# Layer 2's first products by Strassen's scheme: two token tiles and two weight blocks together

## The reference, cut to what matters

```python
h = x @ w_in
g = np.where(h >= 1, h, np.where(h <= -1, 0.0, (h + 1) ** 2 / 4))   # layer 1
x = g @ w_out
h = x @ w_in2                                                       # layer 2
r = np.maximum(h, 0.0)
y = (r * r) @ w_out2
```

## Time and profile before

| what | us |
|---|---|
| median of 3 runs (977.24 to 977.39) | 977.29 |
| span of the profiled execution, first to last instruction | 975.8 |
| what lies around the span, by the median | 1.5 |
| PE busy | 962.4 (99% of the span) |
| DVE busy | 601.0 (62%) |
| ACT busy | 430.9 (44%) |
| POOL busy | 42.0 (4%) |

### The profile page before, as it was taken

One profiled execution on the slowest core, in us unless ns is written; L12 is line 12 of the kernel. 1 busy time (PEld: TensorE's weight loads), 2 busy tenths in 40 slices (PEclk: granted clock), 3 DMA queues, 4 the chain that ended last, 5 costly groups with the idle time before them and its releaser, 6 DMA issues.

```text
span 975.8 us, 22918 instructions
## 1 busy us (share of the span) xinstructions
PE 962.4 (99%) x9520; PEld 781.8 (80%) x9520; DVE 601.0 (62%) x1480; ACT 430.9 (44%) x735; POOL 42.0 (4%) x59
## 2 busy tenths in 40 slices
PE   8899999999999999999999999999999999999998
PEld 7688788777877877787778888888888888888887
DVE  7789888787978787889647763434334334333332
ACT  6667543453455435544545553333333333333333
POOL 5810000000000000000000000000000000000000
PEclk9999999999999999999999999999999999999999
DMA  8252131113012201110004411010010010000000
GB/s 261 81 174 67 59 119 48 27 38 91 35 34 73 71 21 33 49 55 2 2 20 155 162 33 65 1 65 1 1 65 1 0 65 1 33 1 1 33 1 32
DMA packets 28838, 50.65 MB, mean 52 GB/s; under 512 B 2368, under 2 KB 17728, under 8 KB 28736
## 3 DMA queue, kind: packets, MB, share of 16 engines
q1 hardware_dynamic: 28736, 49.19, 15.4%
HBM read 39.75 MB, written 9.44 MB: 50 GB/s over the span
## 4 chain that ended last, share of the span: by engine, by line
PE 87%; DVE 5%; ACT 5%; DMA 2%; issue 1%; SPq 1%; DVEq 0%; ACTq 0%
PE psum L1354 37%; PE psum L1330 37%; PE psum L1077 2%; PE psum L1163 2%; PE psum L1102 1%; PE psum L1214 1%; DVE act_g L1659 1%; ACT kn_sb L804 1%; PE psum L1221 1%; DMA ring<-in_v_s 1%; PE psum L1028 1%; PE psum L1246 1%; ACT act_g L890 1%; DVE diag L1476 1%; ACT u_sb L814 1%
## 5 line engine op out<-in xcount | busy, mean ns | idle before, releaser
L1330 PE MATMUL psum<-x_hi,w 128*128 128x512 f32 x1152 | 390.1, 394 | 0.0
L1354 PE MATMUL psum<-g_hi,w 128*128 128x512 f32 x1152 | 389.7, 393 | 0.0
L1330 PEld LDWEIGHTS psum<-x_hi,w 128*128 128x128 f32 x1152 | 216.1, 188 | 48.9
L1354 PEld LDWEIGHTS psum<-g_hi,w 128*128 128x128 f32 x1152 | 216.1, 188 | 48.4 <-issue 1.8
L1665 DVE TENSOR_TENSOR g_lo<-act_g,g_hi 128x512 fp32r<-128x512 f32 x192 | 132.3, 689 | 159.7 <-ACT g_hi L903 158.6
L1354 PE MATMUL psum<-g_lo,w 128*128 128x512 f32 x576 | 224.3, 389 | 0.0
L903 ACT ACTIVATE g_hi<-act_g 128x512 fp32r<-128x512 f32 x192 | 121.3, 632 | 232.8 <-PE psum L1354 170.6
L1330 PE MATMUL psum<-x_lo,w 128*128 128x512 f32 x576 | 224.0, 389 | 0.0
L1659 DVE TENSOR_TENSOR act_g<-act_g 128x512 f32<-128x512 f32 x96 | 66.4, 691 | 112.1 <-ACT act_g L896 112.1
L1354 PEld LDWEIGHTS psum<-g_lo,w 128*128 128x128 f32 x576 | 108.2, 188 | 21.4
L1330 PEld LDWEIGHTS psum<-x_lo,w 128*128 128x128 f32 x576 | 108.2, 188 | 21.3
(11 more groups left out here) (148 smaller groups left out, 622.0 us busy)
## 6 DMA issues: line engine op xcount, KB each, us to landing
kt_sb<-in_k_t SPq DMA_DIRECT2D x24, 256.0 KB, 4.2
qt_sb<-in_q_t SPq DMA_DIRECT2D x23, 256.0 KB, 3.3
ring<-in_v_s SPq DMA_DIRECT2D x24, 192.0 KB, 3.0
between_layers<-y_out SPq DMA_DIRECT2D x6, 768.0 KB, 4.4
x_sb<-between_layers SPq DMA_DIRECT2D x6, 768.0 KB, 5.6
result<-y_out SPq DMA_DIRECT2D x5, 768.0 KB, 3.9
gram_or_states<-in_k_s SPq DMA_DIRECT2D x15, 192.0 KB, 2.4
wi_st<-in_w_in SPq DMA_DIRECT2D x7, 384.0 KB, 3.6
```

Of the source, the lines that this page charges most:

```text
L1330: ins = pe.matmul(h_ps[n % 2][:, :], w_in_part(layer, f // GW, part)[:, kt, fs], x[:, kt, :], start=(at == 0), stop=(at == len(terms) - 1))
L1354: ins = pe.matmul(acc[kt][:, :], w_out_part(layer, f // GW, part)[:, f % GW, ds], g[n % 2][:, :], start=(f == 0 and j == 0), stop=(f == NF ...
```

## The change

Layer 2 is redone in quads: two token tiles and two hidden blocks together (24 quads: 3 pairs of tiles, 8 weight groups). Of the features' three blocks, the first two are multiplied by a Strassen scheme (7 block products instead of 8) and the third plainly (4), so the four h blocks of a quad come from 11 block products instead of 12. The sums and differences that it needs are made ahead: for x nine combinations per pair of tiles (five sums by POOL in `x2_sums`, nine high parts by ACT in `x2_part`, nine low parts by POOL in `x2_lows`), and for the weights ten blocks of 128 columns per group (`combine_weights` and `low_weights` on POOL, `high_weights` on ACT), plus the 768 columns of the second weights as before. Two of the combined products serve several h blocks; ACT copies the first from PSUM bank 0 to SBUF (`part_u`), DVE makes `part_w` and `part_t` from it and bank 1, and three of the four h blocks leave PSUM by a DVE addition or subtraction, after which ACT's Relu reads SBUF. `combined` is the helper that issues three matmuls per pair, adding to what the bank holds where its last argument is False. Layer 1's steps keep their arithmetic. The diff, cut to its core:

```diff
+        def stage2_of(g):
+
+            return (0, g // 2 + 1) if g in (0, 2) else (1, {1: 1}.get(g, g - 1))
...
+            def load_weights2(g):
+                at = stage2_of(g)[0]
+                if g == 1:
+                    sp.wait_ge(x2_lo_ready, X_COMBOS)
+                elif g:
+                    sp.wait_ge(w2_lo_ready, 2 * (g - 1 if g in (2, 3) else g))
+                cols = slice(g * GW * P, (g + 1) * GW * P)
+                sp.dma_start(plain_in(g).rearrange("p k f m -> p k (f m)"), w_in2.rearrange("(k p) f -> p k f", p=P)[:, :, cols]
+                             ).then_inc(w2_loaded[at], 16)
+                sp.dma_start(combos(g)[:, RAW1:RAW2 + 1, :],
...
+            attention_over()
+            load_raw(0)
+            load_weights2(0)
             store_between(NTT - 2)
-            for g in range(2, NG):
-                load_weights(1, g, w_in2, w_out2)
-                if g == 3:
-                    load_between(0)
-                    load_between(1)
+            for g in range(1, 4):
+                load_weights2(g)
             store_between(NTT - 1)
-            for t in range(NTT):
-                if t + 2 < NTT:
-                    load_between(t + 2)
-                if t < NTT - 1:
-                    store_out(t)
+            for g in range(4, NG):
+                load_weights2(g)
+            load_raw(1)
...
+            def combine_weights(g):
+
+                at, turn = stage2_of(g)
+                pool.wait_ge(w2_loaded[at], 48 * turn)
+                c, w = combos(g), plain_in(g)
+                pool.tensor_tensor(c[:, DIFF, :], w[:, 0, 1, :], w[:, 1, 1, :], ALU.subtract).then_inc(w2_combined, 1)
+                pool.tensor_tensor(c[:, THIRD, :], w[:, 2, 0, :], w[:, 2, 1, :], ALU.add).then_inc(w2_combined, 1)
+                pool.tensor_tensor(c[:, SUM2, :], w[:, 0, 0, :], w[:, 0, 1, :], ALU.add).then_inc(w2_combined, 1)
+                pool.tensor_scalar(c[:, NEG0:NEG2 + 1, :], w[:, :, 0, :], -1.0, None, ALU.mult).then_inc(w2_combined, 1)
+                pool.wait_ge(w2_combined, 6 * g + 1)
+                pool.tensor_tensor(c[:, SUM3, :], w[:, 0, 0, :], c[:, DIFF, :], ALU.add).then_inc(w2_combined, 1)
+                pool.wait_ge(w2_combined, 6 * g + 5)
+                pool.tensor_tensor(c[:, CROSS, :], w[:, 1, 0, :], c[:, SUM3, :], ALU.subtract).then_inc(w2_combined, 1)
+
+            def low_weights(g):
+
+                for out_part, cols in enumerate((slice(0, IN_COLS), slice(IN_COLS, ALL_COLS))):
+                    pool.wait_ge(w2_hi_ready, 2 * g + out_part + 1)
+                    pool.tensor_tensor(w2[g][:, LOW, cols], staged2(g)[:, cols], w2[g][:, HIGH, cols].bitcast(F32),
+                                       ALU.subtract).then_inc(w2_lo_ready, 1)
...
+            def high_weights(g):
+
+                at, turn = stage2_of(g)
+                act.wait_ge(w2_loaded[at], 48 * turn)
+                act.wait_ge(w2_combined, 6 * (g + 1))
+                if g == NG - 1:
+                    act.wait_ge(h_done, STEPS)
+                elif g:
+                    act.wait_ge(mm2_done, first_of(NTT - 1) + GW * (free_for_w2(g) + 1))
+                for cols in (slice(0, IN_COLS), slice(IN_COLS, ALL_COLS)):
+                    act.activation(w2[g][:, HIGH, cols], staged2(g)[:, cols], ACT.Copy).then_inc(w2_hi_ready, 1)
...
+            def drain2(pair, tok):
+                act.wait_ge(out_stored, 16 * (NTT + 2 * pair + tok))
+                last = pair == TOK_PAIRS - 1 and tok == 1
+                if not last:
+                    act.wait_ge(block_done, blocks_by(NG * (pair + 1) - 1, 3 if tok else 2))
+                for kt in range(KT):
+                    if last:
                         act.wait_ge(tail_done, kt + 1)
...
+            def block_high(q, b):
+                act.wait_ge(square_ready, blocks_by(q, b))
+                wait(act, block_done, blocks_by(q - 1, b))
+                act.activation(quad_hi[b][:, :], quad_act(b)[:, :], ACT.Copy).then_inc(quad_hi_ready, 1)
...
+                    if f in (8, 11, 13, 15):
+                        high_weights((8, 11, 13, 15).index(f))
...
+            def quad(q):
+                pair, g = divmod(q, NG)
+                following = pair + 1 if g == NG - 1 and pair + 1 < TOK_PAIRS else None
+                if q:
+                    block_high(q - 1, 3)
+                act.wait_ge(u_done, q + 1)
+                wait(act, w_part_ready, q)
+                if q == 0:
+                    act.wait_ge(w2_lo_ready, 6)
+                act.activation(part_u[:, :], bank[0][:, :], ACT.Copy).then_inc(u_part_ready, 1)
+                if g == 1 and pair:
+                    drain2(pair - 1, 1)
+                if following:
+                    x2_part(following, 0)
+                    x2_part(following, 1)
+                act.wait_ge(c11_done, q + 1)
+                if q:
+                    act.wait_ge(quad_lo_ready, blocks_by(q - 1, 2))
+                else:
+                    act.wait_ge(g_lo_ready, STEPS - 1)
+                act.activation(quad_act(0)[:, :], bank[0][:, :], ACT.Relu).then_inc(relu_ready, 1)
+                if q == 0:
+                    drain(NTT - 1)
+                block_high(q, 0)
+                if following:
+                    x2_part(following, 2)
+                    x2_part(following, 3)
+                if q < 4:
+                    high_weights(q + 4)
+                act.wait_ge(c00_ready, q + 1)
+                block_relu(1)
+                if following:
+                    x2_part(following, 4)
+                block_high(q, 1)
+                act.wait_ge(c10_ready, q + 1)
+                block_relu(2)
+                if following:
+                    x2_part(following, 5)
+                    x2_part(following, 6)
+                block_high(q, 2)
...
+            def u_product(q):
+                if q < NG:
...
+                combos_of_x(q, 1)
+                if q:
+                    pe.wait_ge(c01_ready, q)
+                else:
+                    pe.wait_ge(g_act_ready, STEPS - 1)
+                combined(q, 0, ((DIFF, 0),), True).then_inc(u_done, 1)
...
+            def c11_products(q):
+                combos_of_x(q, 8)
+                pe.wait_ge(u_part_ready, q + 1)
+                combined(q, 0, ((RAW1, 2), (RAW2, 7)), False).then_inc(c11_done, 1)
+
+            def t_products(q):
+                pe.wait_ge(w_part_ready, q + 1)
+                combined(q, 1, ((NEG2, 5), (NEG0, 3)), True).then_inc(t_part_done, 1)
+
+            def c00_product(q):
+                pe.wait_ge(relu_ready, blocks_by(q, 0))
+                combined(q, 0, ((CROSS, 4),), True).then_inc(c00_done, 1)
+
+            def c10_products(q):
+                pe.wait_ge(t_part_ready, q + 1)
+                combined(q, 1, ((THIRD, 5), (SUM2, 6)), False).then_inc(c10_done, 1)
+
+            def c01_products(q):
+                combos_of_x(q, 9)
+                pe.wait_ge(c00_ready, q + 1)
+                combined(q, 0, ((NEG1, 8), (NEG2, 7)), False).then_inc(c01_done, 1)
...
+                    elif b < 2 and g == 0:
+                        pe.wait_ge(acc_ready, KT * (NTT + 2 * pair - 1 + b))
...
+            def first_quad():
+                u_product(0)
+                second_product(STEPS - 2)
+                w_product(0)
+                c11_products(0)
+                second_product(STEPS - 1)
+                t_products(0)
+                c00_product(0)
+                c10_products(0)
+                c01_products(0)
+
+            def quad(q):
+                u_product(q)
+                block_output(q - 1, 0, 0)
+                block_output(q - 1, 0, 1)
+                w_product(q)
+                block_output(q - 1, 0, 2)
+                block_output(q - 1, 1, 0)
+                c11_products(q)
+                block_output(q - 1, 1, 1)
+                t_products(q)
+                block_output(q - 1, 1, 2)
+                block_output(q - 1, 2, 0)
+                c00_product(q)
+                block_output(q - 1, 2, 1)
+                c10_products(q)
+                block_output(q - 1, 2, 2)
+                c01_products(q)
+                for kt in range(KT):
+                    block_output(q - 1, 3, kt)
 
...
+            def block_square(q, b):
+                dve.wait_ge(relu_ready, blocks_by(q, b))
+                dve.tensor_tensor(quad_act(b)[:, :], quad_act(b)[:, :], quad_act(b)[:, :], ALU.mult).then_inc(square_ready, 1)
+
+            def block_low(q, b):
+                dve.wait_ge(quad_hi_ready, blocks_by(q, b))
+                wait(dve, block_done, blocks_by(q - 1, b))
+                dve.tensor_tensor(quad_lo[b][:, :], quad_act(b)[:, :], quad_hi[b][:, :].bitcast(F32), ALU.subtract
+                                  ).then_inc(quad_lo_ready, 1)
+
+            def quad(q):
+                if q:
+                    block_low(q - 1, 3)
...
+                dve.wait_ge(t_part_done, q + 1)
```

(103 more changed lines are left out.)

391 lines of the change are left out of this document (223 added, 168 removed).

## The result

The changed kernel takes 999.74 us (median of 4 runs, 999.18 to 1001.1) beside 977.34 us for the kernel before: a ratio of 1.0233, interval 1.0219 to 1.0247. It is slower, as forecast, but by 22.4 us and not by 7, and it lies above the range of 979 to 992.

The account below looks back on a forecast made before the run. The prediction took PE's matmuls, without a hole in layer 2, as the bound. Its terms, -16.3 + 0.65 + 14.2 + 4.5 + 4.0 = +7.0 us, gave 984.3 us, with a range of 979 to 992.

Parts of the forecast that it names:

- What goes away: Layer 2: 3 matmuls fewer in each of 24 quads, 72 in all at 0.2267 us, 16.3 us off the path.
- A quad in the steady state: Layer 2's steady quads: 15.64 us each on PE, neither ACT nor DVE the bound, so no charge.
- the slack of 1.1 us: Steady quad: c01 leaves its PSUM bank at 14.5 us, PE wants bank 0 again at 15.64; the smallest slack.
- The large hole: End of quad 0: PE waits for c01's subtraction, held up by group 4's store, load and preparation; 14.2 us in the sum.
- Turn of a pair: Quads 9 and 17: PE waits 2.25 us for a bank whose copy waits for `y_out`'s store; 4.5 at two turns.
- The end: After the last matmul: both tiles of the pair end together, so a store precedes the last copies; 4.0 us more.
- The weights before quad 0: POOL and ACT prepare groups 0 to 3 during layer 1; 2.0 to 2.1 us per combination, group 3's high part done at 579.8.
- my upper bound of 2.9: POOL's combination of one weight group: 2.9 us if each small instruction costs the 0.395 of a 256-column copy.
- The lower bound of 1.8: POOL's combination of one weight group: 1.8 us if small instructions cost only their share.
- The first rival: POOL and DVE keep each other waiting everywhere, also in quads 1 to 3: +4 more, 988 us; chance 0.30.
- the weights' turn beyond a quad: Rival, quads 0 to 3: preparing a group takes 16.1 us, longer than a quad; 988 to 991 us; chance 0.10.
- the pace: Rival, layer 2: matmuls start faster than every 226.7 ns; at half the gap 11 us less, 973; chance 0.06.

Follow-up runs that it names:

- the kernel that asks later: Changed kernel with ACT making the high parts of weight groups 4 to 7 one quad later, in quads 1 to 4: 986.03 us.
- The filling experiments: Changed kernel plus unread matmuls in quad 0, 20 ahead of c11 and 60, then 74, behind c01: 1000.99 us, then 997.83.

## Why the prediction was right in sign and wrong in size

**Right.** *What goes away*: 16.3 us, in whole. *A quad in the steady state*: no wait in 78 us, so the slack of 1.1 us covers it. *The large hole*: 14.2 forecast, 14.9 measured, with the chain's links as told (7 us later), and the kernel that asks later loses 12.5 us of it. *Turn of a pair*: 1.93 us idle each for 2.25. *The end*: 4.3 for 4.0.

**Wrong, first: POOL's small instructions** (*The weights before quad 0*). I priced 128 columns by their share of a large instruction, 0.30 us, and the scaling of 384 columns at 0.5, by a one-operand instruction of another kind. They take 0.45 to 0.47 us (one 0.86), also with DVE idle (599.35), and 1.17 to 1.65. Six instructions are 3.4 to 3.8 us, beyond even my upper bound of 2.9, whose floor of 0.395 I had at hand in the earlier trace rows and set aside. (The lower bound of 1.8 doesn't come out of my prices: small ones at their share make 1.5 + 0.5 = 2.0, the forecast itself.) Over four groups this moved `part_u` from 580.45 to 585.7, and PE lost 5.05 us in place of 0.3. Layer 1's last copies, the store and the load come 7 us later (592.73 for 585.75): some 4.75 by this, 1.7 by the slow matmuls behind the hole and 0.3 by layer 2's start.

**Wrong, second: the clock.** The sum has holes of 20 us and not one term for what PE does behind a hole. The trace of before shows layer 2 without a hole and its clock at 1.00, so the price stood in no row; it was still to be bounded, and I didn't name it. It is 6.1 us in this trace (1.7, 2.7, 1.7). The filling experiments show the cause, and that the 2.7 behind the large hole can be had back.

**Wrong, third: the lock, charged at one place only.** I took the full wait in quad 0, where it came about as told (2.23 and 1.53 us), and nothing elsewhere, "where a slack of 1.1 us covers it". In quads 1 to 3 and at the first turn DVE's late c01 subtraction cost 2.7 us; that the lock made all of it is read from DVE's lengthened instructions there (1.3 to 1.8 us beside POOL's low parts and sums), and no run took POOL's work away. The first rival said 4 for it, and was nearer. A slack had been laid out with DVE at 0.69 us; two instructions at up to 2 us use it up.

The three are 4.75 + 6.1 + 2.7 = 13.6 of the 15.1 that the sum fell short; the rest is small (0.5 in quad 0, 0.7 in the large hole, 0.3 at the start and the end each, -0.3 at the turns). Of the rivals, the weights' turn beyond a quad did not happen in quads 1 to 3 (u waited for DVE, not for weights), and the pace did not change.

## What to carry to other kernels

Saving matmuls on a kernel that TensorE bounds pays in full in the steady state; the bill comes at the seams, where lists written for one order meet a load, a store or a shared buffer. There, charge each hole of about 2 us or more twice, once for itself and once for the slow matmuls behind it. A new job on an idle engine is priced instruction by instruction at its floor, with what it does to its neighbour's instructions; and a request that may have to wait goes behind all that doesn't need it: here one moved call was worth 13.7 of the 22.4 us, and with the stores split and the groups later the scheme came out 0.4 to 0.5% ahead.

## What the runs showed of the hardware

- The granted clock falls to the 1.2 GHz level behind a short idle time of PE. Holes of 2.26, 2.35, 2.83, 3.64, 4.05, 5.05 and 14.9 us all did it, for about 8 to 13 matmuls each; 1.86 and 0.53 did not. The turn's hole of 1.90 to 1.93 us comes in twelve places of seven profiled executions (the changed kernel's, and six of the experiments'): nine are followed by slow matmuls, three are not. The changed kernel so has a turn that costs 2.2 us in one place and 3.8 in another.
- POOL with two SBUF operands and DVE with two shut each other out: beside POOL's additions DVE's 0.69 us became 2.7 on the mean. POOL's memsets and DVE's instructions with a PSUM operand are free of it. 64.5 us of such POOL work cost 23.6 us.
- POOL's instructions have a floor: 0.46 us for 128 columns with two operands, where 768 columns took 1.82; a scaling of 384 columns takes 1.17 to 1.65 us.
